# Second layers by pairs of units: Strassen's seven products for the first product's inner block, in a memory map of their own

## The chip, the core and the metric

The kernel runs on one core of a Trainium2 chip. TensorE (PE) multiplies, VectorE (DVE), ScalarE (ACT) and GpSimd (POOL) do the elementwise work, SyncE (SP) issues most transfers. The metric is the device time of one execution in microseconds, lower is better.

## The reference

```python
state = alpha_t[:, None] * state + k_t v_t^T        # per batch (4), head (8), 768 steps, 48 x 48
y_t = q_t @ state
x = y as (3072 tokens, 384)
x = relu(x @ w1_in)**2 @ w1_out                     # 384 -> 2048 -> 384
h = x @ w2_in; out = (h * sigmoid(h)) @ w2_out      # 384 -> 2048 -> 384
```

All is fp32. The weights of the two layer blocks are inputs of the kernel.

## The kernel before, in words

Tokens are cut into 6 units of 512 (128 positions of each of 4 batches). Activations stand with features on partitions, so a tile is 128x512. Each fp32 product is made of three matmuls in fp32r: with a = a_hi + a_lo, the terms w_hi x_hi, w_hi x_lo and w_lo x_hi. For each operand ACT makes the high part (a copy with rounding) and DVE or POOL the low part (raw minus high).

A *step* F is one block f (of NF = 16) of 128 hidden features of one unit. `first_product` (L839) multiplies 3 blocks of 128 inputs into one PSUM bank, `h_ps[f % 2]`: 9 matmuls. ACT reads the bank (`step`, L1067 silu in the second layers, L1069 relu in the first), then makes the high part (L1072), DVE the low part (`low_g`, L1360). `second_product` (L853) of the step LAG = 2 earlier accumulates into three banks `z_ps`: 9 matmuls. F runs from 0 to 191: units 0 to 5 are the first layers of all tokens (steps 0 to 95), units 6 to 11 the second layers (steps 96 to 191). The attention of the later pairs of heads runs beside steps 0 to 76. The last unit's second product is done after everything else as `last_product` (L871), with tokens on partitions: 4 x 16 x 3 matmuls of 384 columns.

After a first-layer unit ACT copies the three `z_ps` banks (`copy_z`, L1085) and SP stores them to `z_scratch`; for a second-layer unit SP loads 768 KB of it into `x_raw`, and ACT and DVE split it. After a second-layer unit DVE transposes the banks (`turn_z`, L1371) and SP stores them in 16 transfers. The second layers' weights come through a ring `w_ring`, loaded from POOL's queue, and are split in steps 80 to 95 by ACT (L1021) and DVE (L1347), two chunks of 128x384 a step.

There is no scheduler: each engine's program is written out, an engine runs its instructions in order, and waits on semaphores are counts of what other engines have done. `h_made`, `act_made`, `g_lo_made`, `z_step` and `z_part` count products, read banks, low parts and second products; a bank is written again when its reader has counted.

## Time and profile before

| | us |
|---|---|
| median of 3 runs | 898.56 |
| lowest, highest | 898.47, 899.72 |
| span of the profiled execution | 896.3 |
| PE busy in it | 883.2 |
| DVE, ACT, POOL busy | 417.9, 399.3, 66.2 |

Busy is the time with at least one instruction running; a matmul is shown with its whole latency, so neighbours overlap. "PEclk" in the windows is the granted clock of PE as a share of the upper level (2.4 GHz; 0.50 is 1.2 GHz). A line of the timeline with "[2.44 <-X]" had the engine idle for 2.44 us before it, until X released it.

### The profile page before, as it was taken

The numbers are of one execution on the slowest core, as the hardware profiler recorded it, in microseconds if no ns is written. First come the engines' busy times: TensorE is split into PE (matmuls) and PEld (weight loads), VectorE is DVE, ScalarE is ACT, GpSimd is POOL, SyncE is SP. The second block draws the span as 40 slices with busy tenths as digits, with TensorE's granted clock in tenths as the row PEclk, the third lists the DMA queues.
The fourth block names the chain that finished last, engine by engine and source line by source line (L and its number), as shares of the span: only waits on it lengthen the run. The fifth ranks groups of instructions, "written<-read, shape, count | busy, mean of one in ns | idle before, by whom it ended". The sixth has DMA issues, their size and how long they took to land.

```text
span 896.3 us, 17305 instructions
## 1 busy us (share of the span) xinstructions
PE 883.2 (99%) x6906; PEld 724.8 (81%) x6906; DVE 417.9 (47%) x907; ACT 399.3 (45%) x710; POOL 66.2 (7%) x97
## 2 busy tenths in 40 slices
PE   7999989999999999999999999999999999999998
PEld 6777768788887887888888888888888888888898
DVE  7688876777767667662443312212212212212310
ACT  4765644455445445543756533323233323233520
POOL 2454300000000000001133000000000000000000
PEclk9999999999999999999999999999999999999999
DMA  9895434333333323311323200200200101100100
GB/s 159 217 244 126 92 72 116 67 79 101 72 89 89 94 66 77 89 22 51 123 90 100 77 1 1 71 0 3 69 1 35 37 1 36 36 0 1 37 11 29
DMA packets 106233, 60.02 MB, mean 67 GB/s; under 512 B 56416, under 2 KB 99808, under 8 KB 106144
## 3 DMA queue, kind: packets, MB, share of 16 engines
q1 hardware_dynamic: 100784, 51.84, 24.3%
q0 software_dynamic: 2048, 6.29, 2.3%
q10 hardware_dynamic: 3312, 0.69, 0.6%
q8 instruction: 57, 0.93, 0.5%
q14 instruction: 32, 0.26, 0.1%
HBM read 45.02 MB, written 9.44 MB: 61 GB/s over the span
## 4 chain that ended last, share of the span: by engine, by line
PE 94%; DVE 3%; issue 1%; ACT 1%; DMA 1%; ACTq 0%; DVEq 0%
PE h_ps L839 42%; PE z_ps L853 40%; PE jobs L871 3%; PE jobs L714 1%; PE jobs L747 1%; PE jobs L816 1%; PE jobs L725 1%; PE jobs L824 1%; PE z_ps L871 1%; DVE decay L1253 1%; PE h_ps L653 1%; PE jobs L703 1%; DMA nat_q<-in_q 1%; PE z_ps L785 0%; DVE decay L1238 0%
## 5 line engine op out<-in xcount | busy, mean ns | idle before, releaser
L1360 DVE TENSOR_TENSOR g_lo<-g,g_hi 128x512 fp32r<-128x512 f32 x177 | 121.5, 687 | 334.0 <-ACT g_hi L1072 242.9
L839 PE MATMUL h_ps<-x_hi,win_hi 128*128 128x512 f32 x576 | 227.1, 394 | 1.3 <-ACT g L1069 0.8
L839 PE MATMUL h_ps<-x_hi,win_lo 128*128 128x512 f32 x576 | 224.4, 390 | 0.0
L839 PE MATMUL h_ps<-x_lo,win_hi 128*128 128x512 f32 x576 | 224.2, 389 | 0.0
L1067 ACT ACTIVATE g<-h_ps 128x512 f32<-128x512 f32 x96 | 57.5, 599 | 232.0 <-PE h_ps L839 232.0
L1069 ACT ACTIVATE g<-h_ps 128x512 f32<-128x512 f32 x96 | 57.4, 597 | 178.6 <-PE h_ps L839 176.4
L839 PEld LDWEIGHTS h_ps<-x_hi,win_hi 128*128 128x128 f32 x576 | 108.1, 188 | 25.1 <-POOL win_lo L592 1.2
L839 PEld LDWEIGHTS h_ps<-x_hi,win_lo 128*128 128x128 f32 x576 | 108.1, 188 | 22.8
L839 PEld LDWEIGHTS h_ps<-x_lo,win_hi 128*128 128x128 f32 x576 | 108.2, 188 | 21.7
L853 PE MATMUL z_ps<-g_hi,wout_hi 128*128 128x512 f32 x288 | 117.3, 407 | 0.0
L1072 ACT ACTIVATE g_hi<-g 128x512 fp32r<-128x512 f32 x177 | 111.8, 632 | 5.6
L853 PE MATMUL z_ps<-g_lo,wout_hi 128*128 128x512 f32 x288 | 112.8, 392 | 0.0
L853 PE MATMUL z_ps<-g_hi,wout_lo 128*128 128x512 f32 x288 | 112.7, 391 | 0.0
L853 PE MATMUL z_ps<-g_hi,win_hi 128*128 128x512 f32 x240 | 93.4, 389 | 0.0
L853 PE MATMUL z_ps<-g_lo,win_hi 128*128 128x512 f32 x240 | 93.4, 389 | 0.0
L853 PE MATMUL z_ps<-g_hi,win_lo 128*128 128x512 f32 x240 | 93.4, 389 | 0.0
L853 PEld LDWEIGHTS z_ps<-g_hi,wout_hi 128*128 128x128 f32 x288 | 54.2, 188 | 12.6
L853 PEld LDWEIGHTS z_ps<-g_hi,wout_lo 128*128 128x128 f32 x288 | 54.3, 189 | 11.8
L853 PEld LDWEIGHTS z_ps<-g_lo,wout_hi 128*128 128x128 f32 x288 | 54.4, 189 | 10.3
L1075 ACT ACTIVATE g<-g 128x512 f32<-128x512 f32 x96 | 59.2, 616 | 0.0
L853 PEld LDWEIGHTS z_ps<-g_lo,win_hi 128*128 128x128 f32 x240 | 45.1, 188 | 9.4
L853 PEld LDWEIGHTS z_ps<-g_hi,win_lo 128*128 128x128 f32 x240 | 45.1, 188 | 9.3
(155 smaller groups left out, 838.9 us busy)
## 6 DMA issues: line engine op xcount, KB each, us to landing
z_scratch<-z_sb SPq DMA_DIRECT2D x18, 256.0 KB, 2.7
x_raw<-z_scratch SPq DMA_DIRECT2D x6, 768.0 KB, 4.6
v_sb<-in_v SPq DMA_DIRECT2D x44, 96.0 KB, 3.0
out_x<-z_sb SPq DMA_DIRECT2D x80, 48.0 KB, 1.7
nat_a<-in_alpha SPq DMA_DIRECT2D x40, 88.0 KB, 2.2
nat_k<-in_k SPq DMA_DIRECT2D x40, 88.0 KB, 2.5
nat_q<-in_q SPq DMA_DIRECT2D x40, 88.0 KB, 2.4
nat_a<-in_alpha SPq DMA_DIRECT2D x40, 80.0 KB, 2.6
```

The source lines that it names most:

```text
L653: last = nc.tensor.transpose(ps[0:ROWS, tile(b)], two, ident[:])
L703: last = nc.tensor.matmul(job_ps[1 + h][:, tile(b)], kp[n % 2][r, tile(b)], qp[n % 2][r, tile(b)], start=True, stop=True)
L714: last = nc.tensor.matmul(job_ps[1 + h][half * HALF:(half + 1) * HALF, b * HALF:(b + 1) * HALF], kp[n % 2][r, cols], qp[n % 2][r, cols], s ...
L725: last = nc.tensor.matmul(job_ps[1 + h][half * HALF:(half + 1) * HALF, at:at + HD], kp[n % 2][r, cols], ident[r, r], start=True, stop=True ...
L839: last = nc.tensor.matmul(h_ps[f % 2][:], w[:, f, tile(kk)], x[par][:, kk, :], start=(kk == TILES[0] and n == 0), stop=(kk == TILES[-1] an ...
L853: last = nc.tensor.matmul(z_ps[m][:], w[:, f, tile(m)], x, start=(f == 0 and n == 0), stop=(f == NF - 1 and n == 2), skip_group_check=True)
L871: last = nc.tensor.matmul(token_ps[b][:, 0:DM], x[:, tile(b)], w[:, f, :], start=(f == 0 and n == 0), stop=(f == NF - 1 and n == 2))
L1067: nc.scalar.activation(g[f % 2][:], h_ps[f % 2][:], ACT.Silu).then_inc(act_made, 1)
L1069: nc.scalar.activation(g[f % 2][:], h_ps[f % 2][:], ACT.Relu).then_inc(act_made, 1)
L1072: nc.scalar.activation(high, g[f % 2][:], ACT.Copy if second else ACT.Square).then_inc(g_hi_made, 1)
L1075: nc.scalar.activation(g[f % 2][:], g[f % 2][:], ACT.Square).then_inc(g_made, 1)
L1360: nc.vector.tensor_tensor(low, g[f % 2][:], high.bitcast(F32), ALU.subtract).then_inc(g_lo_made, 1)
```

## The change

The second layers take two units at once (a *couple*, q = 0 to 2) and two blocks of hidden features (a *group*, n = 0 to 23, eight to a couple). With the inputs in three blocks of 128, the first product of a group is 2 x 2 output tiles (C11, C12, C22, C21: unit and feature block) of 3 terms each, 12 products. The first two input blocks form a 2 x 2 by 2 x 2 product of blocks, done by Strassen's scheme in Winograd's form with 7 products; the third block's 4 products are added in the same PSUM banks where they fit (`FACTORS`): P1, P6, P7 are one product, P2, P5, P3, P4 two each, 11 in all, 33 matmuls.

The operands are sums: of weight blocks (T1 to T4 made by POOL in `t_sums`, four 128x128 operations for each j of 8) and of input tiles (S1 to S4 and D3, made by POOL in `x_sums`, five of 128x512 a couple). The 9 tiles T and B of each j and the 10 tiles S and A of each couple are split into high and low; five low parts a couple are POOL's (`low_s`), the rest DVE's. The products are added up after PE: ACT copies P1 and P5 out of their bank (`spread_first`, `spread_second`), DVE adds P6, P2, P3, P7 and P4 out of PSUM and makes two sums in SBUF (`from_bank` and two more). ACT applies silu and the high part to each C tile (`tile_step`), DVE the low part (`low_tile`). All seven products alternate between the two banks `h_ps`.

The second product is cut into *pieces* of three matmuls for one tile and one output block, put behind the products by `pieces_due`, 12 a group, ten pieces late. In the last couple only unit t = 0 has pieces (6 a group); its other unit's tiles are kept for `last_product`. The last two steps of the first layers, six pieces, run in group 0.

The memory of the first layers is reused: each T and V (w2_out) block has a place over weights that the first layers have finished with, so SP loads them when a count of steps allows (`t_free`, `v_free`). V is loaded already in its turned order, three transfers of 128-byte packets a block, in place of the ring. T is split in steps 80 to 94, S in 85 to 95, V block 0 in step 95, blocks 1 to 3 in group 0, two in each group after. The general path, taken when decays are out of range, changes in the same way and isn't run with these inputs.

```diff
+COUPLES = UNITS // 2
+GROUPS = NF // 2
+PRODUCTS = 7
+A11, S2, A12, A13, S1, S4, D3, S3, A23, A22 = range(10)
+SUMS = 10
+B11, B21, B22, B31, B32, T1, T2, T3, T4 = range(9)
+TILES_T = 9
+FACTORS = [[(B11, A11)], [(T2, S2)], [(B21, A12), (B31, A13)], [(T1, S1), (B32, A23)], [(B22, S4), (B32, D3)], [(T3, S3)],
+           [(T4, A22), (B31, A23)]]
+P1, P6, P2, P5, P3, P7, P4 = range(PRODUCTS)
+
+OUT = [(0, 0), (0, 1), (1, 1), (1, 0)]
+C11, C12, C22, C21 = range(4)
+
+U2_AT, C11_AT, U4_AT, C12_AT, U3_AT, C22_AT, C21_AT = range(1, 8)
+T_ORDER = [0, 1, 6, 2, 7, 3, 5, 4]
+V_STEP = {95: (0,)}
+def v_group(n):
+
+    return {0: (1, 2, 3)}.get(n, (2 * n + 2, 2 * n + 3) if n < GROUPS - 1 else ())
...
+LAG_PIECES = 10
+BESIDE_PRODUCT = [1, 2, 4, 6, 8, 10, 12]
+BESIDE_LAST = [1, 2, 3, 4, 5, 6, 6]
+
+
+def pieces_due(n, r):
+
+    last = (COUPLES - 1) * GROUPS
+    base = PIECES - LAG_PIECES
+    if n < last:
+        due = 12 * n + BESIDE_PRODUCT[r] + base
+        return max(due, min(PIECES, BESIDE_PRODUCT[r])) if n == 0 else due
+    return 12 * last + base + 6 * (n - last) + BESIDE_LAST[r]
...
+            def load_v_block(f):
+
+                what, value = v_free(f)
+                if what == "z_sb":
+                    sp.wait_ge(z_out, 48 * UNITS)
+                else:
+                    sp.wait_ge(h_made if what == "win" else z_step, value)
+                for m in range(KD):
+                    sp.dma_start(v_raw[f][:, tile(m)].rearrange("p (j r) -> p j r", j=QUADS),
+                                 w2_out[bass.ts(f, P), :].rearrange("p (j m r) -> p m j r", j=QUADS, m=KD)[:, m]).then_inc(v_arrived[f], 16)
+
...
+            def x_sums(q):
+
+                pool.wait_ge(x_in, 96 * (q + 1))
+                nc.gpsimd.tensor_tensor(pre[S1][:], pre[S3][:], pre[A22][:], ALU.add).then_inc(x_summed, 1)
+                pool.wait_ge(x_summed, 5 * q + 1)
+                nc.gpsimd.tensor_tensor(pre[S2][:], pre[S1][:], pre[A11][:], ALU.subtract).then_inc(x_summed, 1)
+                nc.gpsimd.tensor_tensor(pre[S3][:], pre[A11][:], pre[S3][:], ALU.subtract).then_inc(x_summed, 1)
+                pool.wait_ge(x_summed, 5 * q + 2)
+                nc.gpsimd.tensor_tensor(pre[S4][:], pre[A12][:], pre[S2][:], ALU.subtract).then_inc(x_summed, 1)
+                nc.gpsimd.tensor_tensor(pre[D3][:], pre[A13][:], pre[A23][:], ALU.subtract).then_inc(x_summed, 1)
+
+            def low_s(q, i):
+                pool.wait_ge(s_hi_made, SUMS * q + i + 1)
+                nc.gpsimd.tensor_tensor(s_lo[:, i, :], pre[i][:], s_hi[:, i, :].bitcast(F32), ALU.subtract).then_inc(s_lo_pool, 1)
...
+            def product(n, r):
+
+                q, j = divmod(n, GROUPS)
+                if n == 0 and r < 2:
+                    pe.wait_ge(act_made, STEPS - 1 + r)
+                elif r < 2:
+                    pe.wait_ge(summed, PRODUCTS * (n - 1) + (U3_AT, C21_AT)[r])
+                elif r in (P2, P7):
+                    pe.wait_ge(spread, 2 * n + (1 if r == P2 else 2))
+                else:
+                    pe.wait_ge(summed, PRODUCTS * n + {P5: U2_AT, P3: C11_AT, P4: C12_AT}[r])
+                if q == 0 and r == 0:
+                    pe.wait_ge(t_lo_made, 2 * (t_place(j) + 1))
+                if j == 0:
+                    if r < P3:
+                        pe.wait_ge(s_lo_pool, ON_POOL * q + (1, 2, 4, 5)[r])
+                    if r == P5:
+                        pe.wait_ge(s_lo_made, (SUMS - ON_POOL) * q + 4)
+                    if r == P4:
+                        pe.wait_ge(s_lo_made, (SUMS - ON_POOL) * (q + 1))
+                bank = h_ps[(PRODUCTS * n + r) % 2]
+                for c, (t, x) in enumerate(FACTORS[r]):
+                    for k, (w, y) in enumerate(((t_hi, s_hi), (t_hi, s_lo), (t_lo, s_hi))):
+                        last = nc.tensor.matmul(bank[:], w[j][:, tile(t)], y[:, x, :], start=(c == 0 and k == 0),
+                                                stop=(c == len(FACTORS[r]) - 1 and k == 2))
+                last.then_inc(product_made, 1)
...
+            def second_piece(k):
+
+                n, i, m = piece_of(k)
+                q, j = divmod(n, GROUPS)
+                t, f = OUT[i][0], 2 * j + OUT[i][1]
+                high, low = tile_parts(n, i)
...
+                        pe.wait_ge(redo_made, 1)
+                for c, (w, x) in enumerate(((v_hi, high), (v_hi, low), (v_lo, high))):
+                    last = nc.tensor.matmul(pair_bank(t, m), w[f][:, tile(m)], x, start=(first and c == 0), stop=(final and c == 2),
+                                            skip_group_check=True)
+                if m == KD - 1:
+                    last.then_inc(tile_used, 1)
+                elif final:
...
+            for n in range(COUPLES * GROUPS):
+                for r in range(PRODUCTS):
+                    product(n, r)
+                    while done < pieces_due(n, r):
+                        if done < PIECES:
+                            first_piece(done)
+                        else:
+                            second_piece(done)
+                        done += 1
+            while done < pieces_all():
+                second_piece(done)
...
+            def spread_first(n):
+
+                act.wait_ge(product_made, PRODUCTS * n + P1 + 1)
+                if n == 0:
+                    act.wait_ge(t_lo_made, 2 * GROUPS)
+                else:
+                    act.wait_ge(tile_lo_made, 4 * (n - 1) + C11 + 1)
+                nc.scalar.activation(s_b[0][:], h_ps[(PRODUCTS * n + P1) % 2][:], ACT.Copy).then_inc(spread, 1)
+
+            def spread_second(n):
+
+                act.wait_ge(product_made, PRODUCTS * n + P5 + 1)
+                wait(act, tile_lo_made, 4 * (n - 1) + C22 + 1)
+                nc.scalar.activation(s_b[3][:], h_ps[(PRODUCTS * n + P5) % 2][:], ACT.Copy).then_inc(spread, 1)
+
+            def tile_step(n, i):
+
+                act.wait_ge(summed, PRODUCTS * n + SUM_OF[i])
+                at = s_b[TILE_IN[i]]
+                nc.scalar.activation(at[:], at[:], ACT.Silu).then_inc(silu_made, 1)
+                act.wait_ge(silu_made, 4 * n + i + 1)
+                slot = in_ring(n, i)
+                if slot is None:
+                    if n % GROUPS == 0:
+                        act.wait_ge(s_lo_pool, ON_POOL * COUPLES)
+                        act.wait_ge(s_lo_made, (SUMS - ON_POOL) * COUPLES)
+                elif slot < 4:
+                    act.wait_ge(g_lo_made, STEPS)
+                    act.wait_ge(z_step, STEPS - (0, 2, 1, 0)[slot])
+                else:
+                    act.wait_ge(tile_used, slot - 3)
+                nc.scalar.activation(tile_parts(n, i)[0], at[:], ACT.Copy).then_inc(tile_hi_made, 1)
...
+            for n in range(COUPLES * GROUPS):
+                q, j = divmod(n, GROUPS)
+                ends = j == GROUPS - 1 and q < COUPLES - 1
+                if j == 0 and q > 0:
+                    s_split(q, A23)
+                spread_first(n)
+                if j == 0 and q > 0:
+                    s_split(q, A22)
+                if ends:
+                    s_split(q + 1, A11)
+                if n > 0:
+                    tile_step(n - 1, C21)
+                if ends:
+                    s_split(q + 1, S2)
+                tile_step(n, C11)
+                if n == 0:
+                    copy_z(UNITS - 1, UNITS - 1, UNITS - 1)
+                if ends:
+                    s_split(q + 1, A12)
+                    s_split(q + 1, A13)
+                spread_second(n)
+                if ends:
...
+            def from_bank(n, r, to, other):
+
+                dve.wait_ge(product_made, PRODUCTS * n + r + 1)
+                nc.vector.tensor_tensor(to[:], h_ps[(PRODUCTS * n + r) % 2][:], other[:], ALU.add).then_inc(summed, 1)
...
+            for n in range(COUPLES * GROUPS):
+                q, j = divmod(n, GROUPS)
+                ends = j == GROUPS - 1 and q < COUPLES - 1
+                if j == 0 and q > 0:
+                    low_s(q, A23)
+                    low_s(q, A22)
+                if q > 0 and j == (1 if q < COUPLES - 1 else 2):
+                    turn_pair(q - 1, 1)
+                if n > 0:
+                    low_tile(n - 1, C21)
+                dve.wait_ge(spread, 2 * n + 1)
+                wait(dve, tile_lo_made, 4 * n)
+                from_bank(n, P6, s_b[1], s_b[0])
+                dve.wait_ge(summed, PRODUCTS * n + U2_AT)
+                from_bank(n, P2, s_b[0], s_b[0])
+                if j == 0 and q > 0:
+                    turn_pair(q - 1, 0)
+                low_tile(n, C11)
+                dve.wait_ge(spread, 2 * n + 2)
+                dve.wait_ge(summed, PRODUCTS * n + U2_AT)
+                nc.vector.tensor_tensor(s_b[2][:], s_b[3][:], s_b[1][:], ALU.add).then_inc(summed, 1)
+                if q == 0:
+                    for f in v_group(j):
+                        low_v(f)
+                dve.wait_ge(summed, PRODUCTS * n + U4_AT)
+                from_bank(n, P3, s_b[2], s_b[2])
+                from_bank(n, P7, s_b[1], s_b[1])
+                dve.wait_ge(summed, PRODUCTS * n + U3_AT)
+                nc.vector.tensor_tensor(s_b[3][:], s_b[1][:], s_b[3][:], ALU.add).then_inc(summed, 1)
+                low_tile(n, C12)
+                if ends:
+                    low_s(q + 1, S4)
+                    low_s(q + 1, D3)
+                from_bank(n, P4, s_b[1], s_b[1])
+                low_tile(n, C22)
+                if ends:
+                    low_s(q + 1, S3)
```

How it moves instructions, at three places.

PE before, the beginning of the second layers: the last three matmuls of step 96's first product, and the first three of step 94's second product.

```order
L839 MATMUL h_ps0<-x_hi0,win2_hi 128x512
L839 MATMUL h_ps0<-x_lo0,win2_hi 128x512
L839 MATMUL h_ps0<-x_hi0,win2_lo 128x512
L853 MATMUL z_ps0<-g_hi1,wout_hi 128x512
L853 MATMUL z_ps0<-g_lo1,wout_hi 128x512
L853 MATMUL z_ps0<-g_hi1,wout_lo 128x512
```

PE after, in group 0: the last half of P3 and all of P7, both of the new first product. `s_` are input tiles and sums, `t_` weight tiles and sums of j = 0.

```order
L1173 MATMUL h_ps0<-s_hi,t_hi0 128x512
L1173 MATMUL h_ps0<-s_lo,t_hi0 128x512
L1173 MATMUL h_ps0<-s_hi,t_lo0 128x512
L1173 MATMUL h_ps1<-s_hi,t_hi0 128x512
L1173 MATMUL h_ps1<-s_lo,t_hi0 128x512
L1173 MATMUL h_ps1<-s_hi,t_lo0 128x512
```

Before, nine matmuls of a second product stood between any two first products. Here P7 follows P3 with no piece between, and P4's six matmuls follow P7; the last first-layer pieces stand ahead of P3.

ACT before, from the end of step 95 to step 98: relu and square of `h_ps`, weight chunks, then silu, and the copies of `z_ps` after step 97.

```order
L1072 ACTIVATE g_hi2<-g1 128x512
L1075 ACTIVATE g1<-g1 128x512
L1021 ACTIVATE win2_hi<-w_ring 128x384
L1021 ACTIVATE win_hi<-w_ring 128x384
L1067 ACT_TABLE_LOAD
L1067 ACTIVATE g0<-h_ps0 128x512
L1072 ACTIVATE g_hi0<-g0 128x512
L1067 ACTIVATE g1<-h_ps1 128x512
L1072 ACTIVATE g_hi1<-g1 128x512
L1085 ACTIVATE z_sb<-z_ps0 128x512
L1085 ACTIVATE z_sb<-z_ps1 128x512
L1085 ACTIVATE z_sb<-z_ps2 128x512
```

ACT after: the last splits of S and of V block 0, then group 0.

```order
L1496 ACTIVATE s_hi<-pre8 128x512
L1496 ACTIVATE s_hi<-pre9 128x512
L1500 ACTIVATE v_hi0<-v_raw0 128x384
L1509 ACTIVATE sum0<-h_ps0 128x512
L1521 ACT_TABLE_LOAD
L1521 ACTIVATE sum0<-sum0 128x512
L1533 ACTIVATE ring_hi0<-sum0 128x512
L1443 ACTIVATE z_sb<-z_ps0 128x512
L1443 ACTIVATE z_sb<-z_ps1 128x512
L1443 ACTIVATE z_sb<-z_ps2 128x512
L1515 ACTIVATE sum3<-h_ps1 128x512
L1500 ACTIVATE v_hi1<-v_raw1 128x384
```

The copies of the last first-layer banks now stand between the first tile's high part and the copy of P5 (`sum3<-h_ps1`); before, nothing but silu steps was behind them.

DVE before, steps 95 to 97:

```order
L1360 TENSOR_TENSOR g_lo2<-g1,g_hi2 128x512
L1347 TENSOR_TENSOR win2_lo<-w_ring,win2_hi 128x384
L1347 TENSOR_TENSOR win_lo<-w_ring,win_hi 128x384
L1360 TENSOR_TENSOR g_lo0<-g0,g_hi0 128x512
L1360 TENSOR_TENSOR g_lo1<-g1,g_hi1 128x512
```

DVE after, group 0 (`sum` are the tiles in which the products are added up):

```order
L1858 TENSOR_TENSOR v_lo0<-v_raw0,v_hi0 128x384
L1868 TENSOR_TENSOR sum1<-h_ps1,sum0 128x512
L1868 TENSOR_TENSOR sum0<-h_ps0,sum0 128x512
L1863 TENSOR_TENSOR ring_lo0<-sum0,ring_hi0 128x512
L1958 TENSOR_TENSOR sum2<-sum3,sum1 128x512
L1858 TENSOR_TENSOR v_lo1<-v_raw1,v_hi1 128x384
L1858 TENSOR_TENSOR v_lo2<-v_raw2,v_hi2 128x384
L1858 TENSOR_TENSOR v_lo3<-v_raw3,v_hi3 128x384
L1868 TENSOR_TENSOR sum2<-h_ps0,sum2 128x512
L1868 TENSOR_TENSOR sum1<-h_ps1,sum1 128x512
L1966 TENSOR_TENSOR sum3<-sum1,sum3 128x512
```

The low parts of three V blocks stand between the first sum with P5 and the sum with P3 (`sum2<-h_ps0,sum2`).

## Rows read from the trace of the kernel before

**Rows 1.** The page: span, busy time of PE, chain of what ended last by engine and line.

```profile
span 896.3 us, 17305 instructions
...
PE 883.2 (99%) x6906; PEld 724.8 (81%) x6906; DVE 417.9 (47%) x907; ACT 399.3 (45%) x710; POOL 66.2 (7%) x97
...
PE h_ps L839 42%; PE z_ps L853 40%; PE jobs L871 3%; PE jobs L714 1%; PE jobs L747 1%; PE jobs L816 1%; PE jobs L725 1%; PE jobs L824 1%; PE z_ps L871 1%; DVE decay L1253 1%; PE h_ps L653 1%; PE jobs L703 1%; DMA nat_q<-in_q 1%; PE z_ps L785 0%; DVE decay L1238 0%
```

**Rows 2.** Windows: length, busy us (count) of PE PEld DVE ACT POOL, PEclk, DMA, GB/s.

```profile
600.00:700.00 100.00, 100.00 (x443) 82.81 (x442) 22.32 (x34) 33.59 (x56) 0.00 (x0) 1.00 0.08 24
```

**Rows 3.** Timeline of second layers: start us, us, engine line op out<-in.

```profile
559.90 0.39 PE L839 MATMUL h_ps<-x_hi,win_lo 128*128 128x512 f32 x1
...
560.33 0.60 ACT L1067 ACTIVATE g<-h_ps 128x512 f32<-128x512 f32 x1 [1.25 <-PE h_ps L839]
...
562.17 0.39 PE L839 MATMUL h_ps<-x_hi,win_hi 128*128 128x512 f32 x1
...
566.25 0.39 PE L839 MATMUL h_ps<-x_hi,win_hi 128*128 128x512 f32 x1
```

**Rows 4.** Timeline of ACT around the change from first to second layers.

```profile
495.05 0.60 ACT L1069 ACTIVATE g<-h_ps 128x512 f32<-128x512 f32 x1
...
497.68 1.28 ACT L1067 ACT_TABLE_LOAD   x1
499.13 0.60 ACT L1067 ACTIVATE g<-h_ps 128x512 f32<-128x512 f32 x1 [0.17 <-PE h_ps L839]
499.76 0.63 ACT L1072 ACTIVATE g_hi<-g 128x512 fp32r<-128x512 f32 x1
...
504.38 1.55 ACT L1085 ACTIVATE z_sb<-z_ps 128x512 f32<-128x512 f32 x3
```

**Rows 5.** Timeline of DVE, the low part of the first silu tile.

```profile
500.42 0.69 DVE L1360 TENSOR_TENSOR g_lo<-g,g_hi 128x512 fp32r<-128x512 f32 x1 [1.93 <-ACT g_hi L1072]
```

**Rows 6.** Groups by line, 440 to 880 us: busy us, mean ns of one.

```profile
L1360 DVE TENSOR_TENSOR g_lo<-g,g_hi 128x512 fp32r<-128x512 f32 x96 | 66.3, 691 | 277.9 <-ACT g_hi L1072 242.9 <-ACT g L1075 35.0
...
L1347 DVE TENSOR_TENSOR win_lo<-w_ring,win_hi 128x384 fp32r<-128x384 f32 x30 | 15.3, 551 | 0.0
L1021 ACT ACTIVATE win_hi<-w_ring 128x384 fp32r<-128x384 f32 x29 | 13.5, 509 | 0.0
...
L1371 DVE STREAM_TRANSPOSE z_sb<-z_ps 128x512 f32<-128x512 f32 x15 | 10.0, 707 | 14.2 <-PE z_ps L853 14.2
```

**Rows 7.** Timeline of PE, its longest wait after the start.

```profile
127.08 0.90 PE L714 MATMUL jobs<-qp,kp 48*64 48x64 f32 x32 [2.44 <-DVE y_sb L1340]
```

**Rows 8.** Windows around that wait, columns as in 2.

```profile
124.00:127.00 3.00, 0.64 (x3) 0.19 (x1) 2.79 (x4) 2.43 (x5) 0.00 (x0) 1.00 0.00 0
127.00:128.00 1.00, 0.92 (x45) 0.95 (x48) 0.00 (x0) 0.00 (x0) 0.00 (x0) 0.70 0.00 0
...
130.00:131.00 1.00, 1.00 (x4) 0.76 (x4) 0.65 (x2) 0.39 (x1) 0.00 (x0) 0.59 0.35 80
131.00:132.00 1.00, 1.00 (x9) 0.55 (x7) 0.00 (x0) 0.00 (x0) 0.00 (x0) 1.00 0.89 155
```

**Rows 9.** Timeline of a POOL subtraction and a DVE multiplication beside it.

```profile
44.40 1.02 POOL L592 TENSOR_TENSOR win_lo<-win_raw,win_hi 128x384 fp32r<-128x384 f32 x1
...
44.62 1.35 DVE L1271 TENSOR_TENSOR kp<-kp,decay 112x512 f32<-112x512 f32 x1
```

**Rows 10.** The tile win_lo on POOL: duration ns min/median/max.

```profile
L592 POOL TENSOR_TENSOR win_lo<-win_raw,win_hi x16: 998/1162/1847, 24.7 to 98.9; 128x384 fp32r<-128x384 f32 x16
```

**Rows 11.** DMA: packets from 3 to 15 us; issues, KB each, median us to landing.

```profile
DMA packets 11345, 2.11 MB, mean 176 GB/s; under 512 B 11345, under 2 KB 11345, under 8 KB 11345
...
x_raw<-z_scratch SPq DMA_DIRECT2D x6, 768.0 KB, 4.6
v_sb<-in_v SPq DMA_DIRECT2D x44, 96.0 KB, 3.0
```

**Rows 12.** Chain of what ended last, three of the four token products.

```profile
860.17 24.98 PE jobs L871 x144
```

More of the change, by code:

```diff
@@ new lines, in build @@
+        s_lo = sb("s_lo", [P, SUMS, UT], F32R)
+        t_high(0)
+        t_low(0)
+        keep_pre(keep_lo, "keep_lo1", 1)
+        pre_tile(9)
+        sb("gap0", [P, 32], F32)
+        with ExitStack() as early:
+            t_raw = [sb(f"t_raw{i}", [P, 6 * P], F32, early) for i in range(2)]
+        for i in range(3):
+            s_b[i] = sb(f"sum{i}", [P, UT], F32)
+        z_stage = []
+        for t in (0, 1):
+            with ExitStack() as late:
+                z_stage.append(sb(f"z_stage{t}", [P, KD * UT], F32, late))
+            for i in range(KD):
+                pre_tile(KD * t + i)
@@ L219, in build @@
+        for j in (1, 2, 3, 4):
+            t_high(j)
+        for f in (7, 8, 9, 10):
+            v_high(f)
+        for j in (1, 2, 3, 4):
+            t_low(j)
+        for f in (7, 8, 9, 10):
+            v_low(f)
+        for j in (6, 7, 5):
+            t_high(j)
+        for f in range(7):
+            v_high(f)
+        for j in (6, 7, 5):
+            t_low(j)
+        for f in range(7):
+            v_low(f)
         nat = {n: [x[:, :, 0:2 * 64].rearrange("p b (h d) -> p b h d", h=2) for x in nat_sb[n]] for n in "akq"}
@@ L627, in _ @@
+            t_sums(6)
+            t_sums(7)
+            for q in (1, 2):
+                x_sums(q)
+                for i in range(ON_POOL):
+                    low_s(q, i)
             pool.wait_ge(redo_made, 1)
@@ new lines, in first_piece @@
+            def first_piece(k):
+                F, m = STEPS - LAG + k // KD, k % KD
+                f = F % NF
+                high, low = g_pair(F)
+                pe.wait_ge(g_lo_made, F + 1)
+                for n, (w, x) in enumerate(((wout_hi, high), (wout_hi, low), (wout_lo, high))):
+                    last = nc.tensor.matmul(z_ps[m][:], w[:, f, tile(m)], x, start=False, stop=(f == NF - 1 and n == 2),
+                                            skip_group_check=True)
+                if m == KD - 1:
+                    last.then_inc(z_step, 1)
+                elif f == NF - 1:
+                    last.then_inc(z_part, 1)
@@ L1123, in _ @@
+            for F in range(STEPS):
                 u, f = divmod(F, NF)
-                step(u, f, g_pair(F)[0], u >= UNITS)
-                if u < UNITS:
-                    square_g(f)
+                step(u, f, g_pair(F)[0], False)
+                square_g(f)
                 if F == 0:
@@ L1397, in _ @@
+            for F in range(STEPS):
                 u, f = divmod(F, NF)
-                if f == 1 and UNITS < u:
-                    if u == UNITS + 1:
-                        wait(dve, z_out, 48 * UNITS)
-                    turn_z(u - 1, u - 1, outs(u - 1 - UNITS))
                 jobs_here = beside(F)
```

462 lines of the change are left out of this document (340 added, 122 removed).

## Prediction

> **What bounds the kernel now.** I read the page first, then windows, then timelines. The page gives PE 883.2 of 896.3 us busy, and the chain that ended last lies to 82% on two lines of PE, the first products at L839 and the second ones at L853 [rows 1]. In the second layers a stretch of 100 us has PE busy for 100.00 us at full clock, while DVE has 22 us of work, ACT 34 and POOL none [rows 2]. So PE is the only bound there, and its unit is the distance of two matmuls, not the 0.39 us that one is shown as busy: a step of 18 matmuls begins at 562.17 and the next at 566.25, 4.08 us, 0.2267 us each [rows 3]. ACT begins to read a product 0.43 us after its last matmul began (559.90 to 560.33), so 0.20 us after the place where the next matmul could begin [rows 3]. Inside ACT, and from ACT to DVE, a dependent instruction follows the end of the one before by about 0.03 us (499.13 + 0.60 to 499.76; 499.76 + 0.63 to 500.42) [rows 4, 5].
>
> **What is removed.** Before, the second layers' first product has 96 steps of 9 matmuls, 864. After, it has 24 groups of 33 (seven products of 3 or 6 matmuls: 3, 3, 6, 6, 6, 3, 6), 792. The second product keeps its count (720 of 512 columns and 192 of 384 at the end), and the token products keep their form, so that stretch stays (144 of its 192 matmuls in 25.0 us [rows 12]). 72 matmuls less at 0.2267 us are **-16.3 us**, if PE stays without a wait. The rest is the search for waits.
>
> **The last unit of the first layers (430 to 497 us).** Here two weight chunks a step go away (ACT 0.51 and DVE 0.55 us each [rows 6]) and the splits of T and S come in: at most 128x640 and 128x512 in a step on ACT, scaled from 0.63 us for 128x512 some 1.4 us, beside relu, square and square, 1.8 us: 3.2 of 4.08 us. DVE has 0.69 + 1.55. Both fit. POOL is new in this place: 32 operations of 128x128 and 10 of 128x512 before the first group ends. A 128x384 one took 1.0 us at best [rows 10], so a 128x512 one is 1.33 by scale; for a 128x128 one the bounds are 0.33 (a third) and 1.0 (no scaling at all). Together 24 to 45 us, in a window from about 439 us (six loads of 256 KB issued at 430, and 768 KB land in 4.6 us [rows 11]) to 497. I take it as hidden and nearer 24; if POOL were later than its place, ACT's queue would stop at a split, the relu behind it too, and PE after some 2 us of slack. Nothing for the sum; 0 to 2 us for the range. The T loads and the six x loads replace loads of as many bytes.
>
> **The first group of the second layers.** Let 0 be the end of step 95, 496.9 us (499.13 less 0.20 less 9 matmuls). PE's order, with a first piece of three matmuls (0.68 us) between, gives P1 0 to 0.68, P6 1.36 to 2.04, P2 2.72 to 4.08, P5 5.44 to 6.80, last first pieces to 8.16. Then P3, P7 and P4 follow with nothing between them. ACT: its step 95 begins at -1.85 (495.05 [rows 4]), has three operations, then two splits of S and one of V, and ends at about 1.4; the copy of P1 to 2.0; the table load, 1.28 us [rows 4], is hidden before the silu at 5.0 to 5.6. The copy to ring_hi0 needs the last step of the first layers, seen at 8.36, so 8.36 to 8.99. Then three copies of z_ps, 1.55 us [rows 4], stand ahead of the copy of P5, which is done at 11.1. P3 is over at 9.52, and P7 needs that bank: **PE waits 1.6 us**. P7 runs to 11.8. On DVE the sum with P5 (to 11.8) and three v_lo, each waiting for its ACT copy (0.51) and taking 0.55 [rows 6], end at 13.1, and only then comes the sum with P3, to 13.8. P4 needs that bank: **2.05 us**. Sum **+3.65 us**. Behind these waits stand all later matmuls; nothing covers them. Bounds: 0 if neither copy nor v_lo were in the way, and about 7 if the V blocks are late as well. The group after it finds everything ready.
>
> **The V blocks.** Sixteen blocks, each three transfers of 512 packets of 128 bytes, are issued on SP's queue behind the steps that free their memory; block 3 can go at -4.1 us and is wanted at 11.9. The nearest rows are 11345 packets under 512 B in 12 us, 1536 in 1.6 us, and V loads of 512 packets of 192 B that land after 3.0 us [rows 11]. So a block is there after some 4 to 5 us, against 16 available; later groups want two blocks in 15.6 us. Hidden. It would have to take over 6 us a block, four in a row, to be felt, and each us beyond is a us in the sum.
>
> **A group in the middle.** 69 matmuls, 15.64 us. The tightest chain runs to P5, which stands at 5.44: P1 seen at 0.88, ACT copy to 1.48, silu of the C21 tile of the group before to 2.1, its high part to 2.74, DVE low part to 3.46, sum with P6 to 4.15. Slack 1.29 us. Work per group on ACT is 10 operations of 0.60 to 0.63, some 6.2 us, on DVE 11 of 0.69, 7.6 us [rows 4, 6]. In the last couple a group has 51 matmuls, 11.56 us, and P5 stands at 4.76: slack 0.61. Elsewhere (P6 on the sum with P4, P3, P7, P4) I find 0.4 us or more. So no wait in a usual group.
>
> **Where couples change.** The ten splits of S lie between on ACT, one more silu slot (0.63 us) ahead of the tight chain, so slack 0.6 to 0.7 in groups 7, 8 and 15. Three transposes, 0.707 us each [rows 6], come ahead of the chain in group 9 (2.1 us, partly into idle time: U2 at 5.1 against 5.44) and in group 18, where P5 stands at 4.76: **+0.35 us**. Between 0 and 2 us for all changes.
>
> POOL subtracts beside DVE there. The trace has one such place: a DVE multiplication with two inputs in SBUF took 1.35 us with a POOL subtraction of 1.02 us beside it, against 0.69 for a usual DVE operation [rows 6, 9]. Ten such POOL operations (1.33 us) lie in groups 7 and 15, ten sums in groups where nothing is tight. A full delay on the chain's low part is 0.66 us, at the slack; I take 0 and keep 0 to 1.3 us. The Trainium skill, page "SBUF — State Buffer", section "SBUF: two separate sides", says that DVE with two SBUF inputs and GpSimd take one port pair as an exclusive lock, so that the loser blocks for the whole instruction. The trace agrees for that one row. By the rule at its worst each couple change would lose about 1 us, and the time would be 890 instead of 888.
>
> **The clock.** The trace shows what a wait of PE can cost beyond itself: PE was idle for 2.44 us before 127.08 [rows 7], and from about 127.4 to 130.8 the granted clock was at the lower level, 1.2 GHz (0.70 over one us, then 0.59 in the last partial one), then again 2.4 [rows 8]. Some 3.4 us at half rate lose 1.7 us. The group above has 3.65 us of idleness with one short product in it, more than that case in sum, but each part shorter. I think a drop likelier than none: **+1.7 us**, bounds 0 and 1.7 (twice 1.7 if it falls twice).
>
> **The sum.** 896.3 - 16.3 + 3.65 + 0.35 + 1.7 = 885.7 us of span. Outside the span the runs have 898.56 - 896.3 = 2.3 us; the profiled execution's own time isn't apart from this, and the three runs lie within 0.14%. **887.9 us.**
>
> **Rivals.** (a) *No lower clock.* The first group waits as above or a little less, and the clock stays up, since no single wait is as long as the one of 2.44 us. 886.2; down to 885 with shorter waits. (b) *Small waits in many places.* POOL's operations, the port, a late V block or a chain in the last couple that is 0.3 us tighter than I have it: 3 to 5 us more, 890 to 893. For it speaks that the last couple's slack is 0.6 us over five handovers; against it, that the handovers read 0.03 us. (c) *The chain bounds every group, slower than before.* Place: ACT copy, silu, high, DVE low, sum, ahead of P5. With x us more on this chain the loss is 16 (x - 1.29) + 8 (x - 0.61), beside the 5.35 us from the first group and the clock. Gain and loss meet at x = 1.52; at 1.9 the loss is 20 us more than the forecast's, 908 us. It needs the chain at 5.7 us instead of 4.15, which would be 0.3 us in each of five handovers instead of 0.03. Against it stand [rows 4, 5]; for it only that sums out of PSUM with a second input from SBUF are new in this place. (d) *No change that can be measured*: the same chain with x between 1.42 and 1.59 us, 896.8 to 900.4.
>
> **Chances.** Forecast 0.50; (a) 0.28; (b) 0.14; (c) 0.05; (d) 0.03. A measurement of this kernel tells about 0.2% from no change. Faster by over 0.2% is 0.92, within 0.03, slower 0.05. The range 885.2 to 892.5 takes in the forecast, most of (a) and most of (b).
>
> **What would show it.** Right: 792 matmuls in the new first products against 864 at the second layers' share of L839, two waits of PE between 505 and 511 us, the first released by an ACT copy out of h_ps, the second by a DVE sum, one stretch of lower clock behind them, PE at 100% and 15.6 us a group afterwards, 11.6 in the last eight. Wrong: gaps at each P5 would mean that the chain of rival (c) rules; waits released by a DMA or by v_lo later than group 0 would mean the V blocks; a wait at the first P1 or P5 would mean POOL; matmuls apart by more than 0.227 us at full clock would fell the first term.

## The result, and the profile after

| | before | after |
|---|---|---|
| median, us | 898.56 (7 executions) | 895.20 (7 executions) |
| lowest, highest | 896.44, 900.43 | 892.10, 896.63 |
| span of the profiled execution | 896.3 | 891.6 |

The ratio is 0.996, with a 95% interval of 0.9944 to 0.9976: faster by 3.4 us, where 10.7 were forecast. 895.2 lies above the range of 885.2 to 892.5. The profiled execution took 893.18 us, 1.58 more than its span.

The page of after, against [rows 1]: PE's busy time and one matmul of the new first product.

```profile
span 891.6 us, 17615 instructions
PE 875.2 (98%) x6834; PEld 712.2 (80%) x6834; DVE 540.8 (61%) x1072; ACT 437.7 (49%) x770; POOL 104.1 (12%) x127
L1173 PE MATMUL h_ps<-s_hi,t_hi 128*128 128x512 f32 x264 | 104.5, 396 | 3.2 <-DVE sum L1868 1.8
```

There are 72 matmuls fewer (6834 for 6906), as forecast. But one of the new first product is shown with 396 ns; before, one of L839 in the second layers was shown with 389. The windows say what this is: the busy time of each engine in each stretch, against [rows 2].

```profile
460.00:480.00 20.00, 20.00 (x90) 16.58 (x89) 9.54 (x13) 13.91 (x25) 10.10 (x17) 1.00 0.21 60
600.00:700.00 100.00, 100.00 (x435) 81.37 (x434) 55.32 (x81) 44.40 (x75) 13.99 (x10) 1.00 0.12 32
```

PE is busy all the time at full clock, as before, but 100 us hold 435 matmuls, where they held 443 in [rows 2]. In 460 to 480 us, still in the first layers, with T and S split beside them, it is 90, as before. So matmuls are further apart in the second layers alone, and PE's share of busy time doesn't show it. The beginnings of two groups, of the group ahead of them (j = 0), and of two in the last couple, from the timeline of PE (start, duration, engine, line):

```profile
626.42 0.39 PE L1173 MATMUL h_ps<-s_hi,t_hi 128*128 128x512 f32 x1
...
642.20 0.40 PE L1173 MATMUL h_ps<-s_hi,t_hi 128*128 128x512 f32 x1
...
658.15 0.40 PE L1173 MATMUL h_ps<-s_hi,t_hi 128*128 128x512 f32 x1
...
801.11 0.40 PE L1173 MATMUL h_ps<-s_hi,t_hi 128*128 128x512 f32 x1
...
812.91 0.40 PE L1173 MATMUL h_ps<-s_hi,t_hi 128*128 128x512 f32 x1
```

A middle group takes 15.95 us, not 15.64, and one of the last couple 11.80, not 11.56. That is 0.231 us a matmul. The group with j = 0 takes 15.78, 0.229 us a matmul.

The waits of PE in the second layers (total, times, longest), and the place in the timeline:

```profile
PE h_ps L1173 <- DVE sum L1868: 1.8, 1, 1.8
PE h_ps L1173 <- ACT sum L1515: 1.4, 1, 1.4
```
```profile
505.98 0.39 PE L1173 MATMUL h_ps<-s_hi,t_lo 128*128 128x512 f32 x1
507.75 0.50 PE L1173 MATMUL h_ps<-s_hi,t_hi 128*128 128x512 f32 x1 [1.39 <-ACT sum L1515]
...
508.32 0.40 PE L1173 MATMUL h_ps<-s_hi,t_lo 128*128 128x512 f32 x1
510.49 0.80 PE L1173 MATMUL h_ps<-s_hi,t_hi 128*128 128x512 f32 x1 [1.77 <-DVE sum L1868]
511.08 0.63 PE L1173 MATMUL h_ps<-s_lo,t_hi 128*128 128x512 f32 x1
...
513.58 0.40 PE L1209 MATMUL z_ps<-ring_lo,v_hi 128*128 128x512 f32 x1
```

P7 begins 1.78 us after the matmul before it and P4 2.17 us after its own, in place of 0.23: 3.5 us of delay, one wait released by an ACT copy and one by a DVE sum. The distance behind a restart is 0.34 us at full clock (507.75 to 508.09), 0.11 more than usual. From 510.49 seven distances together are 3.09 us, where a restart at full clock would take 1.7 (0.34 and six times 0.227): 1.4 us for a fallen clock. The granted clock was at its lower level, 1.2 GHz, from 510.1 to 513.5; one us of it in the windows:

```profile
511.00:512.00 1.00, 1.00 (x4) 0.72 (x3) 0.93 (x3) 0.94 (x3) 0.00 (x0) 0.50 0.60 93
```

ACT and DVE beside the two waits:

```profile
505.66 1.55 ACT L1443 ACTIVATE z_sb<-z_ps 128x512 f32<-128x512 f32 x3
507.09 0.61 ACT L1515 ACTIVATE sum<-h_ps 128x512 f32<-128x512 f32 x1
507.57 1.37 ACT L1500 ACTIVATE v_hi<-v_raw 128x384 fp32r<-128x384 f32 x3
```
```profile
507.73 0.69 DVE L1958 TENSOR_TENSOR sum<-sum 128x512 f32<-128x512 f32 x1 [1.26 <-ACT sum L1515]
508.34 1.49 DVE L1858 TENSOR_TENSOR v_lo<-v_raw,v_hi 128x384 fp32r<-128x384 f32 x3
509.75 1.28 DVE L1868 TENSOR_TENSOR sum<-h_ps,sum 128x512 f32<-128x512 f32 x2
```

These are the queues of the forecast: three copies of `z_ps` (1.55 us) ahead of P5's copy, three low parts of V (1.49 us) between the two sums.

**The account.** From the first matmul of the second layers to the first of the token product it was 363.12 us before (496.89 to 860.01) and is 358.54 after (496.60 to 855.14): 4.58 less. Forecast: -16.3, +3.65, +0.35, +1.7, so -10.6. Seen: the same -16.3, +3.5 of waits, +0.2 of two restarts, +1.4 of clock, and 4.58 fits only if some 6.6 us more are somewhere. The distances are that: 0.31 us in each of 14 middle groups, 0.24 in the eight of the last couple, 0.13 in groups 0 and 8, where j = 0: 6.5 us. The experiments begin with them.

### The profile page after: what moved, and what is told of

It is laid out like the page before. It is cut to its first block, busy times and chain, and to the rows that moved or that the text cites. A ratio compares the mean times of both kernels' runs of the same rounds, so it can differ in the third digit from the quotient of the medians.

```text
span 891.6 us, 17615 instructions
## 1 busy us (share of the span) xinstructions
PE 875.2 (98%) x6834; PEld 712.2 (80%) x6834; DVE 540.8 (61%) x1072; ACT 437.7 (49%) x770; POOL 104.1 (12%) x127
## 4 chain that ended last, share of the span: by engine, by line
PE 93%; DVE 3%; issue 1%; ACT 1%; DMA 1%; ACTq 0%; DVEq 0%
PE z_ps L1144 21%; PE h_ps L1173 21%; PE h_ps L1130 20%; PE z_ps L1209 11%; PE jobs L1209 7%; PE jobs L1229 3%; PE jobs L1005 1%; PE jobs L1038 1%; PE jobs L1107 1%; PE jobs L1016 1%; PE jobs L1115 1%; PE h_ps L1229 1%; DMA nat_k<-in_k 1%; DVE decay L1700 1%; PE jobs L994 1%
## 5 line engine op out<-in xcount | busy, mean ns | idle before, releaser
L1427 ACT ACTIVATE g<-h_ps 128x512 f32<-128x512 f32 x96 | 57.4, 598 | 178.9 <-PE h_ps L1130 176.8
L1521 ACT ACTIVATE sum<-sum 128x512 f32<-128x512 f32 x96 | 60.6, 631 | 140.7 <-DVE sum L1868 117.3
L1868 DVE TENSOR_TENSOR sum<-h_ps,sum 128x512 f32<-128x512 f32 x120 | 82.8, 691 | 61.1 <-PE h_ps L1173 58.2
L1130 PE MATMUL h_ps<-x_hi,win_hi 128*128 128x512 f32 x288 | 115.1, 399 | 1.3 <-ACT g L1427 0.8
L1130 PE MATMUL h_ps<-x_hi,win_lo 128*128 128x512 f32 x288 | 112.3, 390 | 0.0
L1130 PE MATMUL h_ps<-x_lo,win_hi 128*128 128x512 f32 x288 | 112.1, 389 | 0.0
L1173 PE MATMUL h_ps<-s_hi,t_hi 128*128 128x512 f32 x264 | 104.5, 396 | 3.2 <-DVE sum L1868 1.8
L1173 PE MATMUL h_ps<-s_hi,t_lo 128*128 128x512 f32 x264 | 104.8, 397 | 0.0
L1173 PE MATMUL h_ps<-s_lo,t_hi 128*128 128x512 f32 x264 | 104.0, 394 | 0.0
L1863 DVE TENSOR_TENSOR ring_lo<-sum,ring_hi 128x512 fp32r<-128x512 f32 x80 | 56.0, 700 | 69.4 <-ACT ring_hi L1533 69.2
```

The lines of the kernel that those rows point to most:

```text
L1130: last = nc.tensor.matmul(h_ps[f % 2][:], w[:, f, tile(kk)], x[par][:, kk, :], start=(kk == TILES[0] and n == 0), stop=(kk == TILES[-1] an ...
L1173: last = nc.tensor.matmul(bank[:], w[j][:, tile(t)], y[:, x, :], start=(c == 0 and k == 0), stop=(c == len(FACTORS[r]) - 1 and k == 2))
L1427: nc.scalar.activation(g[f % 2][:], h_ps[f % 2][:], ACT.Relu).then_inc(act_made, 1)
L1521: nc.scalar.activation(at[:], at[:], ACT.Silu).then_inc(silu_made, 1)
L1863: nc.vector.tensor_tensor(low, s_b[TILE_IN[i]][:], high.bitcast(F32), ALU.subtract).then_inc(tile_lo_made, 1)
L1868: nc.vector.tensor_tensor(to[:], h_ps[(PRODUCTS * n + r) % 2][:], other[:], ALU.add).then_inc(summed, 1)
```

## The experiments

Spans are a poor measure here, at both ends. The start of the second layers differs by up to 2.4 us between executions (495.44 to 497.79 in kernels with the same code ahead of it). And the last output transfer on ACT's queue took 1.7 us to land in before, after, e2 and e9, but 3.0 to 3.7 us in e1, e3, e4, e5, e7 and e8; this is its row in e1 (KB, us):

```profile
out_x<-z_stage ACTq DMA_DIRECT2D x1, 96.0 KB, 3.7
```

So segments are compared: first matmul of the second layers to first of the token product. e5, e7, e8 and e9 are single executions.

### The spacing: waits and PSUM reads, or the memory map

Two pieces of PE's timeline in after, each from the first matmul of a product of three to the last of the piece behind it: group 8 (j = 0), and group 10 (j = 2).

```profile
632.61 0.39 PE L1173 MATMUL h_ps<-s_hi,t_hi 128*128 128x512 f32 x1
...
633.75 0.39 PE L1209 MATMUL jobs<-ring_hi,v_lo 128*128 128x512 f32 x1
...
661.62 0.39 PE L1173 MATMUL h_ps<-s_hi,t_hi 128*128 128x512 f32 x1
...
662.79 0.40 PE L1209 MATMUL z_ps<-ring_hi,v_lo 128*128 128x512 f32 x1
```

Both run instructions of the same kind. The five distances are 1.14 us in group 8 and 1.17 in group 10. By the starts in ns, group 8 has 226 or 227 ns nearly everywhere and only two longer ones, 233 and 230 or 231, at each change between a product and a piece; group 10 has anything from 224 to 241 ns, inside products too. What differs is where T is. In the memory map S and T0 stand ahead of `gap0`, the 32 floats (128 bytes) that the change puts in; T1 to T7, V and the ring stand behind it. So within group 8's products the weights and the tensor that streams have starts that differ by a multiple of 256 bytes, in group 10's by 128 more. In the kernel before, all sizes ahead of these tensors are multiples of 512 bytes.

**e1: the gap moved ahead of S.** Nothing else.

```diff
+        sb("gap0", [P, 32], F32)
         s_hi = sb("s_hi", [P, SUMS, UT], F32R)
...
-        sb("gap0", [P, 32], F32)
```

> The changed kernel with the 128-byte gap of its memory map moved from behind S and T0 to ahead of them, so that all operands of the second layers' matmuls stand at the same offset modulo 512 bytes (S and T0 were 128 bytes off T1 to T7, V and the ring). No instruction, wait or order is changed. Theory A (the lengthening from 226.67 to 231 ns a matmul comes from the offset between the tensor that streams and the weights loaded meanwhile): a middle group takes 15.64 us again in place of 15.95, the sum over the second layers is 6.6 us, span 891.6 to 885.0. Rival B (it comes from the waits and counts that now stand every three to six matmuls, or from DVE and ACT reading PSUM beside PE): group still 15.95 us, span 891.6 within 0.3.

**e2: the kernel before, moved by 128 bytes.** No instruction is changed here either.

```diff
+        bound = sb("bound", [ROWS, UNITS * PAIRS], F32)
+        all_held = sb("all_held", [ROWS, 1], F32)
         x_raw = sb("x_raw", [P, KD, UT], F32)
...
-        bound = sb("bound", [ROWS, UNITS * PAIRS], F32)
...
-        all_held = sb("all_held", [ROWS, 1], F32)
```

> The kernel before, with two small tensors (128 bytes together) placed ahead of the x and g tiles in place of behind the weights, so that x, g and the second layers' w2_in stand 128 bytes off w1_in, w1_out and the place that w2_out goes to. No instruction is changed. Theory A (offset): both products of the first layers and the second product of the second layers get longer distances, by 2 to 5 ns a matmul on 2500 matmuls or more, 5 to 13 us more than 896.3. Rival B (waits or PSUM reads): 226.67 ns as before, 896.3 within 0.3.

The windows of e1 first, then those of e2, and last the kernel before at 200 to 300 us:

```profile
600.00:700.00 100.00, 100.00 (x443) 82.81 (x442) 56.39 (x83) 45.29 (x76) 13.96 (x10) 1.00 0.12 32
```
```profile
200.00:300.00 100.00, 100.00 (x1159) 79.07 (x1158) 68.46 (x167) 50.25 (x89) 0.00 (x0) 1.00 0.35 89
600.00:700.00 100.00, 100.00 (x434) 81.21 (x433) 22.15 (x33) 32.64 (x55) 0.00 (x0) 1.00 0.06 16
```
```profile
200.00:300.00 100.00, 100.00 (x1167) 80.22 (x1166) 69.94 (x174) 50.81 (x91) 0.00 (x0) 1.00 0.38 90
```

e1 has 443 matmuls, the number of the kernel before. e2 has 434 for 443, and 1159 for 1167 of all kinds in 200 to 300 us. In time: e1 is at 0.9887 of before (0.9869 to 0.9905), 889.26 us against 899.35; its segment is 352.50, 6.04 us less than after's. e2 is at 1.0119 (1.0103 to 1.0136), 909.66 us; its segment is 370.50, 7.4 us more than before's, and it begins 4.1 us later. Theory A's forecast holds both ways, and rival B, which gave no change for either, has fallen: e1 keeps each instruction, each wait and each PSUM read. In e1 the small tensors and the gap ahead of S add up to no multiple of 256 bytes, so it is enough that the starts are alike. A middle group of e1, from its first matmul to the next group's:

```profile
656.80 0.39 PE L1173 MATMUL h_ps<-s_hi,t_hi 128*128 128x512 f32 x1
...
672.45 0.39 PE L1173 MATMUL h_ps<-s_hi,t_hi 128*128 128x512 f32 x1
```

That is 15.64 us (15.65 by the rounded starts), the forecast's number, and so it is in all fifteen. The span of e1 is 888.7 and not 885.0. Of these 3.7 us, its second layers began 1.2 later, and its last output transfer took 2.0 longer (3.7 for 1.7). In the segment, 0.56 us less was gained than the 6.6 expected: the fallen clock cost 0.2 more than in after, and 0.35 us of small waits at P5 of groups 16 and 18, mostly hidden behind the slower matmuls in after, came out (these groups take 11.68 and 11.81 us, the others of the last couple 11.56).

### How far apart, and in which steps

**e5 and e7: the same with 32 and 256 bytes** (`all_held` alone moved; `bound`, `held`, `all_held` and `ones` moved).

> The kernel before with 32 bytes ahead of the x and g tiles in place of behind the weights: x, g and the second layers' w2_in stand 32 bytes off the other weights. Reading 1 (any offset that is not a multiple of 512 costs what 128 costs): some 11.6 us more of span than 896.3, distances of 232 ns in the first layers. Reading 2 (the cost grows with the offset): a quarter, some 3 us. Reading 3 (32 bytes share a 64-byte word with the rest): nothing, 896.3.

> The same kernel with 256 bytes instead. Reading 1 (any offset but a multiple of 512 costs what 128 costs): 11.6 us more than 896.3. Reading 2 (the cost grows with the offset): over 20 us more. Reading 4 (what matters has a period of 256 bytes): nothing, 896.3 and 226.67 ns.

The windows of e5, then of e7:

```profile
600.00:700.00 100.00, 100.00 (x436) 81.42 (x435) 22.18 (x33) 33.12 (x56) 0.00 (x0) 1.00 0.06 17
```
```profile
600.00:700.00 100.00, 100.00 (x443) 82.82 (x442) 23.00 (x35) 33.88 (x56) 0.00 (x0) 1.00 0.08 24
```

256 bytes cost nothing: segment 363.12, as before to the last digit, 898.88 us against 899.19 beside it (the span, 897.3, holds a last transfer 1.6 us longer than before's). 32 bytes cost about as much as 128, not a quarter and not nothing. But the likeness of the spans, 908.1 and 907.9, is in part chance: e5 had no stretch of low clock at 127 us, which e2 had, and a last transfer 1.3 us longer. Its segment is 368.60, 5.5 us more than before's, where e2's is 7.4 more, and in the first layers (430 to 495 us) its mean distance is 233.3 ns, where e2 has 232.4. So reading 1, with its period of 512, fell with e7, readings 2 and 3 with e5, and reading 4 stands: offsets of 32 and 128 bytes cost 2 to 3% of a distance, one of 256 nothing. 64 bytes were not tried.

The second layers of e5 and e2 show more. There x and w2_in, the operands of the first product (L839), are moved together; of the second product (L853), g is moved and w2_out isn't. The beginnings of the products in e5, then those of two first products in e2 and of what follows them:

```profile
566.12 0.39 PE L853 MATMUL z_ps<-g_hi,win_hi 128*128 128x512 f32 x1
...
568.22 0.39 PE L839 MATMUL h_ps<-x_hi,win_hi 128*128 128x512 f32 x1
...
570.27 0.39 PE L853 MATMUL z_ps<-g_hi,win_hi 128*128 128x512 f32 x1
```
```profile
567.72 0.39 PE L839 MATMUL h_ps<-x_hi,win_hi 128*128 128x512 f32 x1
...
569.77 0.40 PE L853 MATMUL z_ps<-g_hi,win_hi 128*128 128x512 f32 x1
...
571.88 0.40 PE L839 MATMUL h_ps<-x_hi,win_hi 128*128 128x512 f32 x1
...
573.97 0.39 PE L853 MATMUL z_ps<-g_hi,win_hi 128*128 128x512 f32 x1
```

In e5 nine matmuls of the second product take 2.10 us and nine of the first 2.05, and inside the first product all distances are 226 or 227 ns: within one kernel the product whose two operands are moved alike is fast, and the other slow. In e2 only every other first product is as fast, 2.05 us; those between take 2.09, 232 ns a distance, though their operands are moved alike too. So equal starts within a product were not always enough beside a product with unequal ones; why, the runs don't show.

The Trainium skill, page "SBUF — State Buffer", section "SBUF: two separate sides", says that within the engine side only the port pair shared by GpSimd and DVE causes contention, and that PE never waits on anyone. By that, addresses would cost PE nothing. In e1 against after they cost 4.5 ns a matmul in a middle group (0.31 us by 69), by the place of two operands alone. Here the measurement decides. What in the hardware does it was not found. That it lies between PE's two operands, weights and moving tensor, and not in a change from one tensor to the next or in another engine, is argued from the inside of group 10's products, where neither operand changes its offset, and from e5's two products; e2's slower first products stay open.

### The first group

**e3: another order on ACT and DVE in group 0**, with after's memory map.

```diff
+                if n == 0:
+                    for f in v_group(0):
+                        v_split(f)
+                    spread_second(0)
                 tile_step(n, C11)
                 if n == 0:
                     copy_z(UNITS - 1, UNITS - 1, UNITS - 1)
...
+                if n == 0:
+                    for f in v_group(0):
+                        low_v(f)
+                if n > 0:
+                    low_tile(n, C11)
...
                 from_bank(n, P3, s_b[2], s_b[2])
+                if n == 0:
+                    low_tile(0, C11)
```

The same calls are left out of their old places for n = 0.

> The changed kernel with its memory map as it is; only in the first group the order on ACT and DVE is changed: V blocks 1 to 3 are split while ACT and DVE idle before P5 ends, and ACT copies P5 before the first C11 tile and the last z_ps banks; DVE takes the low part of C11 after the sum with P3. Theory: the waits of 1.8 and 1.4 us shrink to none and 0 to 0.4, and without them the clock does not fall, which gives 1.7 back: span 891.6 to 886.8 (886.5 to 887.2). Rival 1: the clock falls in this place anyway: 888.4. Rival 2: the waits come back in group 1 since DVE and ACT have the same work: 889 to 891.

```profile
PE h_ps L1173 <- DVE sum L1873: 0.2, 1, 0.2
```

This is the whole list of PE's waits in e3's second layers. The clock stays up. The segment is 354.00, 4.54 us less than after's, against 4.8 expected; 890.79 us, 0.9903 of before (0.9887 to 0.992). The span is 889.4, not 886.8, and so in the range of rival 2: the second layers began 1.0 us later than in after, and the last transfer took 1.4 longer. Rival 2 fell all the same, since no wait came back in group 1, and rival 1 by the clock. The V blocks were there in time for the earlier place, and ACT and DVE had been idle there.

**e8 and e9: one half of it each**, from e1. In e8 `spread_second(0)` alone goes ahead of C11's tile; in e9 the V blocks alone.

> From the kernel with the gap ahead of S: only the copy of P5 is put ahead of C11's tile and of the last z_ps banks; V blocks 1 to 3 stay where they were. Theory: P7 has no wait, but P4 waits for the sum with P3, which stands behind the three low parts of V on DVE, until the same time as before: one wait of some 3.1 us in place of 1.4 and 1.8, and the clock falls. No gain over the kernel with the gap (0 to 0.2 us). Rival: P5's copy was the cause of both waits, and with it gone the second is under 1 us: 2 us or more gained, and no fall.

> From the kernel with the gap ahead of S: only the V blocks are split earlier; the copy of P5 stays behind the z_ps banks. Theory: P7 waits 1.4 us as before, P4 0.6 to 0.7. Gain 1.1 us over the kernel with the gap, and, if the clock stays up with 2.1 us of idleness in two parts, 1.5 us more; if it falls, 1.1 us alone.

PE of e9, then of e8:

```profile
507.91 0.50 PE L1173 MATMUL h_ps<-s_hi,t_hi 128*128 128x512 f32 x1 [1.39 <-ACT sum L1515]
...
509.36 0.51 PE L1173 MATMUL h_ps<-s_hi,t_hi 128*128 128x512 f32 x1 [0.49 <-DVE sum L1871]
```
```profile
510.05 0.79 PE L1173 MATMUL h_ps<-s_hi,t_hi 128*128 128x512 f32 x1 [3.89 <-DVE sum L1871]
```

e9: waits of 1.39 and 0.49 us, and no fall of the clock (0.34 us after a restart, then 0.23); segment 349.63, 2.9 us less than e1's, against 2.6 expected. e8: one wait of 3.89 us in place of 3.1, the clock falls (0.59 and then 0.43 us a matmul), and the segment is 354.62, 2.1 us longer than e1's where no change was expected. So the V low parts on DVE were the longer half, and moving the copy alone does harm. Three things were missed. First, ACT's table load of 1.28 us came behind the early copy and pushed C11's tile, the `z_ps` copies and the V blocks back; PE's one delay is 4.06 us, where e1's two cost 3.6 with the restart between them. Second, the granted clock was low from 508.4 to 515.2, 6.8 us in place of the 3.4 in e1 and after, which cost 0.8 us more than in e1. A window of e8 in which it is still low:

```profile
514.00:515.00 1.00, 1.00 (x4) 0.75 (x3) 0.30 (x1) 0.00 (x0) 0.00 (x0) 0.50 0.54 85
```

Third, 30 us later PE waited 0.52 us in a place where it had not waited in after or e1, and the group takes 16.50 us for 15.64. PE, DVE and POOL of e8 there, and DVE in the same place of e1:

```profile
544.58 0.50 PE L1173 MATMUL h_ps<-s_hi,t_hi 128*128 128x512 f32 x1 [0.52 <-DVE sum L1871]
```
```profile
537.38 1.72 DVE L1866 TENSOR_TENSOR ring_lo<-sum,ring_hi 128x512 fp32r<-128x512 f32 x1 [1.36 <-ACT ring_hi L1533]
539.02 1.78 DVE L1961 TENSOR_TENSOR sum<-sum 128x512 f32<-128x512 f32 x1
540.72 3.21 DVE L1861 TENSOR_TENSOR v_lo<-v_raw,v_hi 128x384 fp32r<-128x384 f32 x2
```
```profile
540.21 1.73 POOL L892 TENSOR_TENSOR pre<-pre 128x512 f32<-128x512 f32 x1
541.90 1.60 POOL L893 TENSOR_TENSOR pre<-pre 128x512 f32<-128x512 f32 x1
```
```profile
538.09 0.69 DVE L1863 TENSOR_TENSOR ring_lo<-sum,ring_hi 128x512 fp32r<-128x512 f32 x1 [1.36 <-ACT ring_hi L1533]
539.32 1.16 DVE L1958 TENSOR_TENSOR sum<-sum 128x512 f32<-128x512 f32 x1 [0.54 <-ACT sum L1515]
```

Two low parts of V took 3.21 us on DVE beside POOL's sums, where three took 1.49 us alone, and P3's sum stood behind them. They took the same 3.21 us in after (539.75) and in e1 (540.40), where PE didn't wait. What e8 has beyond that are the two DVE operations ahead of them, 1.72 and 1.78 us beside POOL's sums, where e1 has 0.69 and 1.16. What the prediction's passage on POOL has from the Trainium skill (page "SBUF — State Buffer", section "SBUF: two separate sides"), one port pair as an exclusive lock, agrees with these rows, and it costs PE 0.5 us where the chain happens to meet it; in after the collision (V low parts of 1.64 us at 539.75 and 541.32) met slack.

**e4: both edits.**

> Both edits together: the gap ahead of S, and the new order in the first group. If the two causes are apart, the gains add: 891.6 less 6.6 less 4.8 is 880.2 of span, some 882 to 883 as an execution. If the spacing hid a part of the waits or the other way round, less: 881 to 884 of span.

```profile
600.00:700.00 100.00, 100.00 (x443) 82.81 (x442) 56.33 (x82) 44.97 (x75) 13.94 (x10) 1.00 0.12 32
```

883.16 us, 0.9824 of before (0.9811 to 0.9837), segment 347.68: 10.9 us less than after's and 15.4 less than before's, of 16.3 that the missing matmuls are worth. The two gains add up (6.04 + 4.54 = 10.58; the rest is the clock and spacing of group 0). The span is 881.0 against 880.2 expected, closer than its parts: the second layers began 1.2 us earlier than in after, and the last transfer took 1.6 longer. It beats both kernels. The mean granted clock is 0.998 in all four executions of e4, and 0.994 to 0.996 in the seven of after and the four of e1, so the fall in the first group is not one execution's. What is left is 0.45 us at P4 of group 0 and 0.35 us at P5 of groups 16 and 18.

## Why the prediction was wrong

**Removed matmuls.** This is the term that failed. The count, 72, was right. What was wrong is the price of those that remain: "72 matmuls less at 0.2267 us" takes the distance of the kernel before for all 792 + 720 that remain, in a memory map that the change makes new. It was 0.231 us, and 6.5 us are lost, so 4.58 us came where 10.6 were forecast for the segment. The forecast had named this ("matmuls apart by more than 0.227 us at full clock would fell the first term"), but gave it no rival and no width. The cause was in the change: `gap0`, 128 bytes, between S and most other operands, and "a memory map of their own" was put at nothing without a reason. e1 and e4 give back the 0.2267 and with it 15.64 us a group.

**The first group.** +3.65 forecast, 3.5 seen; P7 on ACT's copy of P5 (1.6, seen 1.55), P4 on the sum with P3 (2.05, seen 1.94). Mechanism, place and sizes right; e3 and e9 confirm the cause.

**The clock.** +1.7, seen 1.4. It fell behind 1.39 and 1.77 us of idleness with three matmuls between (after, e1); in the one execution of e9 it did not behind 1.39 and 0.49. The row that the forecast took it from is less sure than it looked: the first layers' wait near 127 us is 2.3 to 2.4 us long in all ten profiled executions, and the clock fell behind it in eight, not in e5 and e8. The two restarts, 0.11 us each, were not in the sum.

**The last unit, V blocks, POOL.** As forecast: nothing. POOL's 128x128 operation took 0.46 us when alone, its 128x512 one 1.30 (bounds 0.33 to 1.0, and 1.33), and the V blocks were early.

**Middle groups and couple changes.** No wait in a usual group, right. For P5 of group 18 0.35 us was taken. In after the slower matmuls left 0.06 of it; in e1 and e4 it is 0.25, and P5 of group 16 has 0.1.

**Outside the span.** 2.3 us were taken, as the distance of a median from one execution's span; the profiled execution itself has 1.58. This term is 0.7 too large. On the other side the profiled execution of after is among its fastest, 2.0 under the median. So 885.7 + 6.5 - 0.2 (waits) - 0.3 (clock) + 0.2 (restarts) - 0.3 (group 18) is 891.6, the span, and 891.6 + 1.6 + 2.0 is 895.2. The seven executions of after differ by 4.5 us; between profiled executions the start of the second layers and the last transfer differ by 2.4 and 2.0 us, and the cause of either stays open.

Rivals: (a) fell, the clock did drop. The time lies between (b) and (d), by a cause that neither names; (c) and (d) fell, since the chain never held PE in a usual group.
